# Token-major output matmuls, and the query product merged and moved, in an attention and two-network kernel

## The reference

```python
mag = sqrt(a_re**2 + a_im**2); scale = minimum(mag, 0.999) / (mag + 1e-6)
for t in range(S):                      # per batch and head, state D x D
    S_re, S_im = ar*S_re - ai*S_im + outer(k_t, v_t), ar*S_im + ai*S_re
    y_t = q_t @ S_re
x = y as (3072, 384)
x = softplus(x @ w_in) @ w_out          # 384 -> 2048 -> 384
out = ((x @ w1) * (x @ w2)) @ w3 @ w_out2   # 384 -> 1024 -> 1024 -> 384
```

## Time and profile before

| | us |
|---|---|
| median of three runs | 985.9 |
| the profiled execution | 985.9 |
| its span, first to last instruction | 984.1 |
| TensorE busy in the span | 898.6 |
| VectorE busy | 608.6 |
| ScalarE busy | 426.4 |
| GpSimd busy | 70.0 |

### The profile page before, as it was taken

The page is one execution under the profiler, slowest core; times in us unless marked ns, Lnnn a source line. Parts: engine busy times, 40 slices in busy tenths (PEclk is TensorE's granted clock), DMA queues, the critical chain, the costliest instruction groups (busy, mean ns, idle before and its releaser), DMA issues.

```text
span 984.1 us, 14229 instructions
## 1 busy us (share of the span) xinstructions
PE 898.6 (91%) x5298; PEld 800.5 (81%) x5298; DVE 608.6 (62%) x982; ACT 426.4 (43%) x612; POOL 70.0 (7%) x56
## 2 busy tenths in 40 slices
PE   0973739999999999999999999999999999999998
PEld 0543639989989989989889999998888888888887
DVE  5978978989898998898999832355221212121211
ACT  4143263585574674664764654587112020202011
POOL 0000000000000000000000000000222222222221
PEclk9995668999999999999999999999999999999999
DMA  9766065273372381570570550421101010101000
GB/s 336 243 192 192 21 195 130 69 195 99 109 182 74 116 215 36 149 201 13 158 196 12 143 113 13 146 90 47 35 1 65 1 65 1 64 0 64 0 32 33
DMA packets 97878, 99.50 MB, mean 101 GB/s; under 512 B 6928, under 2 KB 88848, under 8 KB 97808
## 3 DMA queue, kind: packets, MB, share of 16 engines
q1 hardware_dynamic: 97808, 98.59, 34.5%
HBM read 63.96 MB, written 29.88 MB: 95 GB/s over the span
## 4 chain that ended last, share of the span: by engine, by line
PE 63%; DVE 21%; ACT 5%; DVEq 5%; issue 3%; DMA 1%; ACTq 1%; SPq 0%
PE ps L1313 8%; PE ps_p L1313 8%; PE ps L1315 8%; PE ps L1314 7%; PE ps_p L1315 7%; PE ps_p L1314 7%; PE ps_ay L1349 3%; DVE sp L1192 2%; DVE an L1018 2%; PE ps_ay L1313 2%; PE ps_ay L1314 2%; PE ps_ay L1315 2%; PE ps_k L1313 2%; PE ps_k L1314 2%; PE ps_k L1315 2%
## 5 line engine op out<-in xcount | busy, mean ns | idle before, releaser
L1313 PE MATMUL ps<-g_h,wo_h 128*128 128x384 f32 x384 | 133.3, 347 | 2.1 <-DVE g_l L1199 2.1
L646 POOL TENSOR_TENSOR abl<-ab,abh 128x512 fp32r<-128x512 f32 x48 | 69.0, 1438 | 907.3 <-DVE abh L1296 907.3
L1315 PE MATMUL ps<-g_h,wo_l 128*128 128x384 f32 x384 | 129.4, 337 | 0.0
L1314 PE MATMUL ps<-g_l,wo_h 128*128 128x384 f32 x384 | 129.2, 336 | 0.0
L1313 PE MATMUL ps_p<-x1h,win_h 128*128 128x384 f32 x336 | 116.9, 348 | 6.2 <-DVE sp L1192 6.2
L1315 PE MATMUL ps_p<-x1h,win_l 128*128 128x384 f32 x336 | 112.6, 335 | 0.0
L1314 PE MATMUL ps_p<-x1l,win_h 128*128 128x384 f32 x336 | 112.5, 335 | 0.0
L1349 PE MATMUL ps_ay<-stq,stk 96*128 96x128 f32 x384 | 55.1, 289 | 37.6 <-DVE am L1141 14.8
L1287 DVE TENSOR_TENSOR ab<-ps_ay,bc 128x512 f32<-128x512 f32 x24 | 16.6, 692 | 114.6 <-ACT bc L914 114.6
L1349 PEld LDWEIGHTS ps_ay<-stq,stk 96*128 96x128 f32 x384 | 52.1, 202 | 40.0 <-issue 25.8
L762 ACT ACTIVATE g_h<-sp 128x768 fp32r<-128x768 f32 (+1 forms) x71 | 55.4, 780 | 66.6 <-DVE sp L1192 66.2
(11 more groups left out here) (160 smaller groups left out, 1992.3 us busy)
## 6 DMA issues: line engine op xcount, KB each, us to landing
qk_scr<-tt SPq DMA_DIRECT2D x16, 576.0 KB, 4.8
stq<-qk_scr SPq DMA_DIRECT2D x48, 192.0 KB, 4.6
qk_scr<-pp SPq DMA_DIRECT2D x16, 576.0 KB, 4.2
stk<-qk_scr SPq DMA_DIRECT2D x48, 192.0 KB, 4.5
an<-in_a_re SPq DMA_DIRECT2D x8, 576.0 KB, 4.0
an<-in_a_im SPq DMA_DIRECT2D x8, 576.0 KB, 5.2
qk<-in_q SPq DMA_DIRECT2D x8, 576.0 KB, 7.6
qk<-in_k SPq DMA_DIRECT2D x8, 576.0 KB, 8.7
```

The source lines that it names most:

```text
L646: tensor_tensor(abl[:, m % AR, :], ab[:, m % 2, :], abh[:, m % AR, :].bitcast(F32), ALU.subtract).then_inc(ab_lo, 1)
L1313: mm(o, wh, xh, start=start, stop=False)
L1314: mm(o, wh, xl, start=False, stop=False)
L1315: return mm(o, wl, xh, start=False, stop=stop)
```

## The change

Four things are edited.

- **down2** keeps a 128-token slice of the activation as the stationary operand and streams 384 columns of w34. A block has 12 matmuls of 384 columns in place of 9 of 512. The result is tokens by channels, in four banks. The fourth is `ps_ay[:, 1]`.
- **out_tile, store and the counts** of o_mm and o_ev go from 3 to 4 per tile. The output tensor is (3072, 384), so a DMA row has 1536 B in place of 2048 B; the last tile is stored in four pieces.
- **The query product** is one VectorE instruction over both parts, with the query broadcast, in step 4 ahead of add_relu. store_q waits once, ahead of both DMAs.
- **keys** goes from after add_relu to before it, in step 5.

```diff
-        ps_o = [ps_2[:, mo, :] for mo in range(G)]
+        ps_o = [ps_2[:, 0, 0:DM], ps_2[:, 1, 0:DM], ps_2[:, 2, 0:DM],
+                ps_ay[:, 1, 0:DM]]
...
+                wait(prep_q, m + 1)
                 if not first:
                     for c in range(NCH):
                         wait(q_rd[c], 32 * m)
                 for i in range(2):
-                    wait(prep_q, 2 * m + i + 1)
                     eng.dma_start(c_p(qk_scr[i]), by_g(tt[:, i, :])).then_inc(q_wr, 16)
...
             def store(t, u):
-                wait(o_ev, G * t + G + G)
-                eng.dma_start(out_c[:, :, bass.ts(t, T2)], ost[:, u, :, :]).then_inc(o_wr[u], 16)
+                wait(o_ev, 4 * t + 4 + 4)
+                eng.dma_start(out[bass.ts(t, T2), :].rearrange("(s p) n -> p s n", p=P),
+                              ost[:, u, :, :]).then_inc(o_wr[u], 16)
...
-            for mo in range(G):
-                wait(o_ev, G * (NT2 - 1) + mo + 1 + G)
-                eng.dma_start(out_c[:, mo, bass.ts(NT2 - 1, T2)], ost[:, 1, mo, :]).then_inc(o_wr[1], 16)
+            for s_ in range(4):
+                wait(o_ev, 4 * (NT2 - 1) + s_ + 1 + 4)
+                eng.dma_start(out[T2 * (NT2 - 1) + P * s_:T2 * (NT2 - 1) + P * s_ + P, :], ost[:, 1, s_, :]).then_inc(o_wr[1], 16)
...
             def out_tile(t, u):
-                for mo in range(G):
-                    eng.wait_ge(o_mm, G * t + mo + 1 + G)
-                    if mo == 0:
+                for s_ in range(4):
+                    eng.wait_ge(o_mm, 4 * t + s_ + 1 + 4)
+                    if s_ == 0:
                         eng.wait_ge(o_wr[u], 8 * t + (16 if u == 0 else 8))
-                    act(ost[:, u, mo, :], ps_o[mo], ACT.Copy).then_inc(o_ev, 1)
+                    act(ost[:, u, s_, :], ps_o[s_], ACT.Copy).then_inc(o_ev, 1)
...
-            def prep_q_(m, i):
-                if i == 0:
-                    eng.wait_ge(qk_ld, 32 * m + 32)
-                ve.tensor_tensor(tt[:, i, :], qk[:, 0, :], pp[:, i, :], ALU.mult).then_inc(prep_q, 1)
+            def prep_q_(m):
+                eng.wait_ge(qk_ld, 32 * m + 32)
+                ve.tensor_tensor(tt[:, :, :], qk[:, 0:1, :].to_broadcast([P, 2, GT]), pp[:, :, :], ALU.mult).then_inc(prep_q, 1)
...
-            after_mask = {0: steps("run", 1), 1: steps("run", 5), 2: steps("carry", 2), 3: by[:2], 4: [("q", 0)], 5: ["inverse"]}
-            after_sum = {0: steps("run", 2), 1: steps("run", 6), 2: steps("carry", 4), 3: by[2:3], 4: [("q", 1), "p2"], 5: ["keys"]}
+            after_mask = {0: steps("run", 1), 1: steps("run", 5), 2: steps("carry", 2), 3: by[:2], 4: ["q"], 5: ["inverse", "keys"]}
+            after_sum = {0: steps("run", 2), 1: steps("run", 6), 2: steps("carry", 4), 3: by[2:3], 4: ["p2"], 5: []}
...
             def down2(t, m):
                 eng.wait_ge(ab_lo, NM2 * t + m + 1 + 2)
-                for mo in range(G):
+                for s_ in range(4):
                     if m == 0:
-                        eng.wait_ge(o_ev, G * t + mo + 1)
-                    ms = slice(P * mo, P * mo + P)
-                    last = mm3(ps_o[mo], w34h[:, m, ms], w34l[:, m, ms], abh[:, m % AR, :], abl[:, m % AR, :],
-                               m == 0, m == NM2 - 1)
+                        eng.wait_ge(o_ev, 4 * t + s_ + 1)
+                    ts = slice(P * s_, P * (s_ + 1))
+                    ah, al = abh[:, m % AR, ts], abl[:, m % AR, ts]
+                    mm(ps_o[s_], ah, w34h[:, m, :], start=m == 0, stop=False)
+                    mm(ps_o[s_], ah, w34l[:, m, :], start=False, stop=False)
+                    last = mm(ps_o[s_], al, w34h[:, m, :], start=False, stop=m == NM2 - 1)
```

More of the change, by code:

```diff
@@ L140, in build @@
         assert at2 <= at_win_l + 4 * G * DFF
-        ost, _ = sb("ost", [P, 2, G, T2], at=at_g)
+        ost, _ = sb("ost", [P, 2, 4, DM], at=at_g)
         ps_p = ctx.enter_context(nc.psum_tensor("ps_p", [P, 2, 512], F32))
@@ L611, in _ @@
                 load_x2_first()
-            out_c = out.rearrange("(g p) t -> p g t", p=P)
             def store(t, u):
-                wait(o_ev, G * t + G + G)
-                eng.dma_start(out_c[:, :, bass.ts(t, T2)], ost[:, u, :, :]).then_inc(o_wr[u], 16)
+                wait(o_ev, 4 * t + 4 + 4)
+                eng.dma_start(out[bass.ts(t, T2), :].rearrange("(s p) n -> p s n", p=P),
+                              ost[:, u, :, :]).then_inc(o_wr[u], 16)
             load_x2(1, 1)
@@ L624, in _ @@
             store(NT2 - 2, 0)
-            for mo in range(G):
-                wait(o_ev, G * (NT2 - 1) + mo + 1 + G)
-                eng.dma_start(out_c[:, mo, bass.ts(NT2 - 1, T2)], ost[:, 1, mo, :]).then_inc(o_wr[1], 16)
+            for s_ in range(4):
+                wait(o_ev, 4 * (NT2 - 1) + s_ + 1 + 4)
+                eng.dma_start(out[T2 * (NT2 - 1) + P * s_:T2 * (NT2 - 1) + P * s_ + P, :], ost[:, 1, s_, :]).then_inc(o_wr[1], 16)
             wait(o_wr[0], 16 * NT2 // 2 + 16)
-            wait(o_wr[1], 16 * NT2 // 2 + 16 + (G - 1) * 16)
+            wait(o_wr[1], 16 * NT2 // 2 + 16 + 3 * 16)
         @block.gpsimd
@@ L658, in _ @@
             eng.sem_inc(x2_ev, G)
-            eng.sem_inc(o_ev, G)
+            eng.sem_inc(o_ev, 4)
             def raw_high(i):
@@ L1076, in prep @@
                         prep_p_(m, even, first)
-                    elif piece[0] == "q":
-                        prep_q_(m, piece[1])
+                    elif piece == "q":
+                        prep_q_(m)
                     elif piece == "p2":
@@ L1159, in _ @@
             raw_low(3)
-            prep(0, True, steps("carry", 8, 16, 32) + by + ["p", ("q", 0), ("q", 1), "p2", "inverse", "keys", "keys end"], first=True)
+            prep(0, True, steps("carry", 8, 16, 32) + by + ["p", "q", "p2", "inverse", "keys", "keys end"], first=True)
             prep(1, False, ["m2", "newton", "scale start", "scale"] + steps("a", 0, 1))
@@ L1176, in _ @@
                     raw_low(7)
-            prep(1, False, steps("q", 0, 1))
+            prep(1, False, ["q"])
             x1_low(0)
@@ L1294, in tile2 @@
                     else:
-                        eng.wait_ge(o_mm, G * t + G)
+                        eng.wait_ge(o_mm, 4 * t + 4)
                     ve.tensor_copy(abh[:, m % AR, :], ab[:, m % 2, :]).then_inc(ab_hi, 1)
@@ L1317, in _ @@
             eng.sem_inc(ab_free, NM2 - 1)
-            eng.sem_inc(o_mm, G)
+            eng.sem_inc(o_mm, 4)
             eng.sem_inc(g_free, 1)
@@ L1552, in tokens_in_order @@
     def tokens_in_order(x):
-        x = np.asarray(x).reshape(DM, B * S // CT, RUN, CT // RUN)
-        return np.ascontiguousarray(x.transpose(1, 3, 2, 0).reshape(B * S, DM))
+        x = np.asarray(x).reshape(B * S // CT, RUN, CT // RUN, DM)
+        return np.ascontiguousarray(x.transpose(0, 2, 1, 3).reshape(B * S, DM))
     arrays = {name: channels_by_tokens(inputs[name]) for name in ("a_re", "a_im", "q", "k")}
@@ L1572 @@
     aps["w34_scr"] = nc.dram_tensor("w34_scr", (NM2, P, DM), F32, kind="Internal").ap()
-    aps["out"] = nc.dram_tensor("out_0", (DM, B * S), F32, kind="ExternalOutput").ap()
+    aps["out"] = nc.dram_tensor("out_0", (B * S, DM), F32, kind="ExternalOutput").ap()
     build(nc, **aps)
```

## The result

The changed kernel takes 1000.97 us, the median of four runs (998.71 to 1001.32), beside 986.56 us (985.79 to 990.23, four runs) for the kernel before: a ratio of 1.0134, interval 1.0104 to 1.0164. In a second comparison it was 1.0112 (1.0095 to 1.0129). It is slower by 11 to 14 us where 7.3 were forecast, above the range.

A forecast was written before the change was run, and what follows sets the result against it. TensorE and VectorE take turns in the first network; TensorE alone bounds the second. Slots +5.6, output matmuls +1.9, tail -0.2 make +7.3 us on 985.9: forecast 993.2 us, range 987.5 to 996.5.

The forecast's parts named there:

- The output matmuls: Second network's down2: 12 matmuls of 384 columns for 9 of 512 add 39 ns per block, 1.9 us over 48.
- rival C: First network: longer stalls bring TensorE's clock down, +5.5 us over three even slots, 998.7 us; chance 0.06.
- Even slots: Slots 0, 2, 4: q's delay passes through TensorE back into VectorE's queue, +1.24 us each, 3.7 us in all.
- The keys' delay is caught again by the end of the slot: Slots 0 to 4: up(7) starts later, but VectorE, relieved of keys behind add_relu(6), recovers the keys' delay by slot end.
- Rival D: Slots: the keys' delay is not caught before the slot's end, 1000.9 us; chance 0.03.
- Odd slots: Slots 1 and 3, walked on n=3: TensorE's idle before the state takes up most delay; +0.25 us each, 0.5 in all.
- Slot 5: Last attention slot, n=5: no later stall swallows the delay of up(7), so all 1.5 us stay.
- The first network in all: Slots and preparations together: 3.7 + 0.5 + 1.5 - 0.1 = +5.6 us, all from waits.
- The tail: Very end of the kernel: earlier last matmul result, shorter eviction and smaller last store gain 0.2 us, bounds 0 to 0.4.
- Rivals A and B: A: VectorE's own queue sets slot ends, 985.6 us, chance 0.06. B: slack hides moves, second network pays, 987.6 us, 0.08.

The follow-up runs named there:

- the stalls filled: Extra matmuls, results unread, where TensorE waits ahead of up(6) and up(7): changed kernel 996.38 us, ratio 1.0079; keys moved alone, filled ahead of up(7), 991.6 us, 1.0026.
- the keys alone: Kernel before with only keys moved ahead of add_relu(6); query product and output part as before: 993.8 us, ratio 1.0052.
- the moves alone: Kernel before with the merged early query product and the earlier keys, without the output part: 994.58 us, ratio 1.0062.
- the output part alone: Changed kernel with query product and keys put back as before, leaving only the down2 and store change: 992.33 us, ratio 1.0045.
- q behind add_relu: Kernel before with the query product merged but placed behind add_relu(5), and ScalarE's two squares moved behind its softplus: 991.17 us, ratio 1.0026.
- the paired order: Output part without the VectorE moves, TensorE order changed to up2, up2, down2, down2: 991.32 us, ratio 1.0023 to the kernel before.
- the nine matmuls: Kernel before with down2 as 9 matmuls of 384 columns, operand roles kept, 128 tokens of each tile left out: 970.59 us in one execution.
- either move alone: Kernel before with only the query product merged ahead of add_relu(5): 991.53 us, ratio 1.0028; or with only keys moved ahead of add_relu(6): 993.8 us, 1.0052.

## Why the prediction was wrong, point by point

**The output matmuls, forecast 1.9 us, measured 5.0: the step that failed most.** "12 x 173.3 - 9 x 226.8 = 39 ns per block" (38.4 as written, 40 with the steady steps of 173.3 and 226.7) took its two steps from streams of one length: the first network has only 384 columns ahead of and in the earlier trace rows, the second had only 512. Both steps are there in the trace after, in the second half of each group, and the 40 ns with them. What the sum left out is that 48 blocks now have two changes of length each, one of about 26 and one of about 41 ns, spread over the next six and nine matmuls: 67 ns x 48 = 3.2 us. The experiments show that it goes with the change of length (halved when the changes are halved, the same with nine as with twelve matmuls) and not with the operands' roles. Why the matmuls behind such a change take longer is open; no row of the trace tells.

The trace of before could have warned. Where the 384-column matmuls of up follow matmuls of 48 columns, a group of eighteen takes 3.22 us and not the 3.12 of eighteen steady steps. TensorE's timeline of before, first, seventh and eighteenth matmul of such a group:
```profile
368.98 0.42 PE L1313 MATMUL ps_p<-x1h,win_h 128*128 128x384 f32 x1
...
370.12 0.34 PE L1313 MATMUL ps_p<-x1h,win_h 128*128 128x384 f32 x1
...
372.03 0.33 PE L1315 MATMUL ps_p<-x1h,win_l 128*128 128x384 f32 x1
```
The first six steps take 1.14 us, 190 ns each, the next eleven 1.91, 173.6. Over 30 such groups the steps are 258, 175, 180, 174, 176, 174, 175 ns and then 173; behind a group of the same length they are 173 from the first on. A group whose first matmul had to wait starts slowly too (280, then 175 to 180 for some five). So the 67 ns are likely one case of something wider than 384 against 512 columns, which no run here took apart. The bounds of 1.3 to 2.5 us covered only the rounding of starts; a mix of lengths that the earlier trace rows doesn't have wanted a bound of its own. An estimate from the Trainium skill's figure (TensorE: Matmul & The Clock Gate, Wait — 56ns, not 53.3ns?), some 2.5 ns of fixed cost per matmul, makes the part 0.4 us; measured were 5.0, and the steady steps alone have 13.3 ns over their columns' 160.0.

**The clock, rival C, forecast a chance of 0.06.** It happens. In the slots of the five traces with unfilled stalls of 1.5 to 2.0 us, 24 such stalls were followed by 8 falls to the 1.2 GHz level: 2 behind the twelve ahead of up(6), of 1.5 to 1.6 us, and 6 behind the twelve ahead of up(7), of 1.9 to 2.0. Each is worth about 1.6 us of TensorE's work, part of which the next stall takes up. In the slots of the nine traces without such stalls, or with the stalls filled, there is none. The argument against C was that TensorE was busier here than in the earlier trace rows; a third of the stalls bring the clock down all the same. C's price of 5.5 us was too high as it was worked out: not three slots each time but one or two, 2.2 us in the slots of both profiled executions; the changed kernel with and without the filling is 0.33% apart, 3 us, by the ratios of two comparisons, which takes in the second network's start. The Trainium skill (same page, HAM oscillation — how this bites in real kernels) has a kernel whose waits in each loop bring the clock down again and again; the rows behind up(6) and up(7) are that, at shorter waits, and not every time.

**Even slots, forecast 1.24 each.** Right in kind: idle before up(6) 1.49 to 1.59 (forecast 1.9), before up(7) 1.87 (2.0), mask(5) 1.99 (2), none before down(6), and add_relu(7) later as it should be. Too large in size: 1.09, 0.91 and 0.72 us with the clock up. The whole of 1.24 was taken as passing through add_relu(5) to the slot's end in each; part of it was slack, more in slot 4 than in 0. In slot 2, against TensorE's work ahead of it, add_relu(5) was 0.98 later and add_relu(7) 0.86, where 1.24 stood for both. "The keys' delay is caught again by the end of the slot" is right: 0 in slots 0, 2 and 4 with the keys alone and the stalls filled. Rival D is out with it.

**Odd slots, forecast 0.25 each.** 0.05 in slot 3, which is near. In slot 1 the change gains 0.32: its add_relu(5) had slack before up(6) (the idle there is 0.32 after), and its wait for the state, 0.60 before, is gone. It was walked on n=3 alone and the result carried to n=1; the walk held for the slot that it was made on.

**Slot 5, forecast 1.5.** 1.28; 1.25 and 1.54 with the keys alone.

**The first network in all.** Waits 3.7 us (5.6 forecast), clock 2.2 in the profiled execution. By accident they come to 5.9, close to the 5.6 that was forecast for other reasons; only the traces with the stalls filled tell the two apart. 0.5 us more was waited at the second network's start, where the wait went from 2.12 to 2.60 us; in the second trace of the changed kernel it is 2.08, and over all traces 2.03 to 2.60, so this is spread between executions and not the change.

**The tail**, forecast -0.2: 3.55 us from the last matmul's start to the end are now 3.29. The evictions are 0.49 us as expected, and the waits around them stayed covered.

**Rivals A and B** are out: up(6) and up(7) are later with each move, and the moves alone cost 0.62%.

**What is chance in the first comparison.** The 2.7 us ahead of up(0, 2), the 0.5 waited at the second network's start, and perhaps the 1.6 of clock there. Against the same unchanged stretch of the profiled run of before, the start-up lags between 0 and 2.9 us in the other traces, without relation to the edit (2.2 with the output part alone, 0 with the keys alone). Since nearly all of them lag by about 2 us, the base of the forecast was itself a lucky one: 985.9 us, where the later medians of the same kernel are 988.02 to 988.93. At the second network's start the clock fell in 6 of 14 traces: in both of the changed kernel, and in those of q behind add_relu, the paired order, the nine matmuls and both moves, but not with the output part alone, either move alone, or the fillings. The wait there was 2.08 us in one in which it fell and 2.43 in one in which it didn't, so the length of the wait alone doesn't decide it. Whether a part of the change makes this likelier is open. The change's own price is best taken from the second comparison, 1.12% or 11 us: 5.0 of steps, 3.7 of waits, less 0.3 at the tail, which make 8.4, and the rest clock: 2.2 us in the slots of each of the two traces, and up to 1.6 at the second network's start. (With the stalls filled, where the 8.4 should stand alone, the medians are 7.5 us apart, and the ratio's interval is 6.5 to 9.2.)

## What to carry to other kernels

Take a matmul's step from a stretch that has the same mix of lengths as the new one; where no row has it, price the alternation apart, and prefer an order that runs equal lengths together. Moving VectorE work ahead of something that TensorE waits for costs its length once if it returns through TensorE into VectorE's own queue, and nothing if the slot's later stalls absorb it, so walk each slot that differs, not one of a kind. A stall that is absorbed later can still cost more than it seems, since TensorE may work at half its clock behind it: look at the granted clock in short windows behind each stall, as the mean (0.959 for 0.967) and the page's slices of 25 us hide this.

## What the runs showed of the hardware

- A change between 384 and 512 moving columns in a stream of 128x128 loads costs about 26 ns (512 to 384, over six matmuls) and 41 ns (384 to 512, over nine); the steps of a steady stream are 173.3 and 226.7 ns. Behind matmuls of 48 columns the first seven of 384 are slow as well (3.22 us for eighteen, 3.12 when steady).
- Stalls of only 1.5 to 2.0 us on a TensorE that is otherwise busy were followed by the 1.2 GHz level in 8 of 24 cases; with 5 to 10 matmuls in each gap the clock stayed at 1.00 in the slots of both traces with the stalls filled.
- Between executions the same unchanged stretch, the first 160 us, differs by up to 2.9 us of 987, a third of a per cent, which one profiled pair can't tell from an edit. The granted clock of the same 20 us in it was 0.50 in one trace and 0.76 in another.
